# Attention half heads before a three-pass MLP: zeros products in the prologue, four q and k buffers, and the half heads' normalising and copying exchanged between ScalarE and VectorE

## The reference, cut to what matters

```python
# attention: B, H, S, D = 4, 8, 576, 64, causal window of 128 keys, ALiBi slope 2**-(h+1)
scores = scale * np.matmul(q, k.transpose(0, 1, 3, 2))
scores = np.where(mask, scores + bias[None], -1000000000.0)
scores = scores - np.max(scores, axis=-1, keepdims=True)
attn = np.exp(scores)
attn = attn / (np.sum(attn, axis=-1, keepdims=True) + 1e-09)
x = np.matmul(attn, v)                        # heads side by side: (4, 576, 512)
# block 1
xn = (x - mu) / np.sqrt(var + 1e-06) * g_ln
x = x + np.maximum(xn @ w_ch1, 0.0) @ w_ch2   # 512 -> 2048 -> 512
# block 2
h = np.maximum(x @ w_in, 0.0)                 # 512 -> 1024
h = h * (1.0 / (1.0 + np.exp(-conv_out)))     # conv_out: 3 taps over the sequence
out = h @ w_out
```

## Time and profile before

| | us |
|---|---|
| median of 3 runs | 871.1 (866.97 to 873.47) |
| the profiled execution | 875.55 |
| its span | 873.8 |
| PE busy | 828.9 (95%) |
| DVE, ACT, POOL busy | 525.8, 365.3, 177.2 |
| first 71.1 us: mean granted clock of TensorE | 0.64 |
| 71.1 to 136.0: the same | 0.79 |
| 182 to the end: the same | 0.99 or more |

### The profile page before, as it was taken

One profiled execution on the slowest core, in us unless ns is written; L12 is line 12 of the kernel. 1 busy time (PEld: TensorE's weight loads), 2 busy tenths in 40 slices (PEclk: granted clock), 3 DMA queues, 4 the chain that ended last, 5 costly groups with the idle time before them and its releaser, 6 DMA issues.

```text
span 873.8 us, 17079 instructions
## 1 busy us (share of the span) xinstructions
PE 828.9 (95%) x5836; PEld 778.6 (89%) x5836; DVE 525.8 (60%) x1444; ACT 365.3 (42%) x1007; POOL 177.2 (20%) x170
## 2 busy tenths in 40 slices
PE   8988878599998999999899999999999999999998
PEld 5556667589997999999899999999999899999998
DVE  3543455668755677764577773631226977888772
ACT  3423334356632365552255652221325444444432
POOL 6334456322201221110111120111111101111100
PEclk8558789999999999999999999999999999999999
DMA  4231343221203112301312311221222022211201
GB/s 125 63 93 55 92 134 93 82 66 51 82 8 116 54 44 69 96 9 55 99 35 63 96 42 56 77 68 43 89 85 83 14 84 75 75 56 46 81 21 41
DMA packets 56110, 59.29 MB, mean 68 GB/s; under 512 B 24800, under 2 KB 43232, under 8 KB 55520
## 3 DMA queue, kind: packets, MB, share of 16 engines
q1 hardware_dynamic: 56032, 58.30, 22.4%
HBM read 44.12 MB, written 14.16 MB: 67 GB/s over the span
## 4 chain that ended last, share of the span: by engine, by line
PE 78%; issue 9%; DVE 8%; ACT 2%; POOL 1%; SPq 1%; DMA 0%; ACTq 0%; POOLq 0%; DVEq 0%
PE bank L1280 21%; PE bank L1282 20%; PE bank L1281 20%; PE bank L1182 3%; PE bank L1206 3%; PE bank L1221 3%; PE bank L1251 3%; PE bank L1235 3%; PE bank L1195 2%; PE bank L1263 1%; PE bank L1173 1%; DVE small L905 1%; DVE prob L912 1%; DVE prob L949 1%; ACT prob L732 1%
## 5 line engine op out<-in xcount | busy, mean ns | idle before, releaser
L1280 PE MATMUL bank<-xn_hi,wa_hi 128*128 128x288 f32 x512 | 159.4, 311 | 3.6 <-DVE xn_lo L1001 2.4
L1280 PE MATMUL bank<-h_hi,wb_hi 128*128 128x288 f32 x512 | 158.4, 309 | 0.5 <-DVE ch_stage L1017 0.5
L1281 PE MATMUL bank<-xn_lo,wa_hi 128*128 128x288 f32 x512 | 154.0, 301 | 0.0
L1282 PE MATMUL bank<-xn_hi,wa_lo 128*128 128x288 f32 x512 | 153.8, 300 | 0.0
L1281 PE MATMUL bank<-h_lo,wb_hi 128*128 128x288 f32 x512 | 152.4, 298 | 0.0
L1282 PE MATMUL bank<-h_hi,wb_lo 128*128 128x288 f32 x512 | 152.1, 297 | 0.0
L1006 DVE SCALAR_TENSOR_TENSOR h_lo<-bank,h_hi 128x288 fp32r<-128x288 f32 x128 | 58.2, 454 | 123.2 <-ACT h_hi L762 121.8
L762 ACT ACTIVATE h_hi<-bank 128x288 fp32r<-128x288 f32 x128 | 52.4, 409 | 186.0 <-PE bank L1282 185.2
L1280 PEld LDWEIGHTS bank<-xn_hi,wa_hi 128*128 128x128 f32 x512 | 98.7, 193 | 7.2 <-issue 4.9
L1280 PEld LDWEIGHTS bank<-h_hi,wb_hi 128*128 128x128 f32 x512 | 97.7, 191 | 3.0 <-issue 1.4
L1281 PEld LDWEIGHTS bank<-xn_lo,wa_hi 128*128 128x128 f32 x512 | 98.9, 193 | 0.0
(11 more groups left out here) (127 smaller groups left out, 1721.8 us busy)
## 6 DMA issues: line engine op xcount, KB each, us to landing
w_stage<-w SPq DMA_DIRECT2D x32, 256.0 KB, 2.9
k_raw<-qkT SPq DMA_DIRECT2D x48, 144.0 KB, 2.9
q_raw<-qkT SPq DMA_DIRECT2D x48, 144.0 KB, 2.9
x_in<-x_spill SPq DMA_DIRECT2D x8, 580.0 KB, 4.2
ch_in<-ch_spill SPq DMA_DIRECT2D x8, 580.0 KB, 5.2
x_spill<-xT SPq DMA_DIRECT2D x4, 1152.0 KB, 4.6
ch_spill<-ch_stage SPq DMA_DIRECT2D x32, 144.0 KB, 1.9
out<-out_stage SPq DMA_DIRECT2D x32, 144.0 KB, 1.8
```

The costliest lines, as they stand in the source:

```text
L1280: nc.tensor.matmul(dst, w_h, a_h, start=start, stop=False)
L1281: nc.tensor.matmul(dst, w_h, a_l, start=False, stop=False)
L1282: last = nc.tensor.matmul(dst, w_l, a_h, start=False, stop=stop)
```

## The change

It does five things.

- **Zeros products.** The 14 at the start become 9. The fours before three heads go; instead 8 stand before the first HP, 4 before each of the six after it, 7 and 10 around the last heads, then 9 before the first OUT, 4 before the second and the third, and 4 before the first product of block 1: 79 instead of 44.
- **Four q and k buffers.** Two more buffers of 2x384 columns lie in the former gaps behind `half_pt0` and `half_pt1`. The loads of heads 2 and 3 are issued at the start, in front of the v loads of heads 1 and 2; each later one waits for the scores of head e - 4.
- **Pads later.** The new buffers lie where the pads of `pt_hi` and `pt_lo` are, so POOL clears these only after the last scores of half 1, in "first", and PE waits for them before the first O of batch 1 and no longer before "first".
- **Normalising on ACT, copying on DVE.** `half_normalise` is now on ACT, a Copy with a scale per row; DVE keeps the sum and the reciprocal as `half_inverse`, and takes `half_pt_copy`.
- **Other times.** In "first" HP comes at 2.2 slots after HS (2.9 before) and HO at 4.3 (5.15 before); the new steps have delays counted from HS. Head 0 of half 1 is normalised between the prologue and "first".

```diff
@@ -88,16 +88,18 @@
-HALF_FIRST = {("HS", 0): 0.0, ("HP", 0): 2.9, ("HO", 0): 5.15}
+HALF_FIRST = {("HS", 0): 0.0, ("HP", 0): 2.2, ("HO", 0): 4.3}
-WARM_START, WARM_HEAD, WARM_NORM = 14, 4, 6
+WARM_START = 9
+WARM = [(1.79, 8)] + [(m + 0.78, 4) for m in range(2, H)] + [(H + 0.3, 4), (H + 0.7, 3), (H + 1.2, 4), (H + 1.7, 6)]
+WARM += [(H + 2.3 + t, n) for t, n in ((0.3, 9), (0.6, 4), (0.9, 4), (1.2, 4))]
...
@@ -158,7 +160,7 @@
-        out += [(n - 0.2, ("WARM", WARM_HEAD)) for n in range(3)] + [(H + 2.3 + t, ("WARM", WARM_NORM)) for t in (0.3, 0.6, 0.9)]
+        out += [(t, ("WARM", n)) for t, n in WARM]
...
@@ -286,9 +288,10 @@
-        sb("half_gap0", [P, PTN - 512], scope=half)
+        half_qk2 = sb("half_qk2", [P, 2, 384], scope=half)
-        sb("half_gap1", [P, PTN - 512 + 2 * S + NT * D], scope=half)
+        half_qk3 = sb("half_qk3", [P, 2, 384], scope=half)
+        sb("half_gap1", [P, 2 * S + NT * D], scope=half)
...
@@ -299,6 +302,8 @@
+        half_qk += [half_qk2[0:D], half_qk3[0:D]]
+        assert PTN - 512 == 768
...
@@ -438,12 +443,12 @@
-                if e >= 2:
-                    c2, h2 = divmod(e - 2, H)
-                    sp.wait_ge(bank_filled, use_of(0, ("HS", c2, h2, len(HGROUPS[c2]) - 1)) + 1)
+                if e >= 4:
+                    c4, h4 = divmod(e - 4, H)
+                    sp.wait_ge(bank_filled, use_of(0, ("HS", c4, h4, len(HGROUPS[c4]) - 1)) + 1)
-                sp.dma_start(half_qk[e % 2][:, :, 0:n], qkT[0, h, :, :, HK0[c]:HK0[c] + n]).then_inc(half_qk_loaded[e % 2], 16)
+                sp.dma_start(half_qk[e % 4][:, :, 0:n], qkT[0, h, :, :, HK0[c]:HK0[c] + n]).then_inc(half_qk_loaded[e % 4], 16)
...
@@ -500,8 +505,10 @@
+            load_half_qk(0, 2)
+            load_half_qk(0, 3)
...
@@ -514,7 +521,7 @@
-                        e = half_no(a[0], a[1]) + 2
+                        e = half_no(a[0], a[1]) + 4
...
@@ -607,10 +614,13 @@
-            nc.gpsimd.memset(pt_hi[:, PTZA:PTN].bitcast(F32), 0.0).then_inc(zeros_ready, 1)
-            nc.gpsimd.memset(pt_lo[:, PTZA:PTN].bitcast(F32), 0.0).then_inc(zeros_ready, 1)
+            def clear_pt_pads():
+                pool.wait_ge(bank_filled, use_of(0, ("HS", 1, H - 1, 0)) + 1)
+                nc.gpsimd.memset(pt_hi[:, PTZA:PTN].bitcast(F32), 0.0).then_inc(zeros_ready, 1)
+                nc.gpsimd.memset(pt_lo[:, PTZA:PTN].bitcast(F32), 0.0).then_inc(zeros_ready, 1)
...
@@ -649,13 +659,15 @@
-                          ("W", 0.3, "w_lo"), ("Y", 1.0, "y"), ("HS", -early, "scale")]
+                          ("W", 0.3, "w_lo"), ("Y", 1.0, "y"), ("HS", -early, "scale"), ("HS", 0.9, "pads")]
+                    elif name == "pads" and a[0] == 1 and a[1] == H - 1:
+                        clear_pt_pads()
...
@@ -714,13 +726,13 @@
-            def half_pt_copy(c, h):
-                e = half_no(c, h)
-                act.wait_ge(bank_filled, use_of(0, ("HP", c, h, 0)) + 1)
-                if e >= 2:
-                    c2, h2 = divmod(e - 2, H)
-                    act.wait_ge(bank_filled, use_of(0, ("HO", c2, h2, 0)) + 1)
-                nc.scalar.activation(half_pt[e % 2][:], bank[bank_of(0, ("HP", c, h, 0))][:], ACT.Copy).then_inc(half_pt_ready, 1)
+            def half_normalise(c, h):
+                e, r = half_no(c, h), half_rows(c, h)
+                act.wait_ge(half_sum, 2 * e + 2)
+                for t in range(HNT[c]):
+                    rows, _, _, keys, _, col = HTILES[c][t]
+                    probs = half_prob_of(c, h)[0:rows, col:col + keys]
+                    nc.scalar.activation(probs, probs, ACT.Copy, scale=row_inv[0:rows, r + t:r + t + 1]).then_inc(half_prob, 1)
...
@@ -787,7 +799,7 @@
-                          ("HS", 0.5, "half_exps"), ("HP", 0.6 if kind == "prologue" else 0.3, "half_pt")]
+                          ("HS", 0.5, "half_exps"), ("HS", 1.85 if kind == "prologue" else 1.1, "half_normalise")]
...
@@ -823,6 +836,7 @@
+            half_normalise(1, 0)
...
@@ -899,17 +913,20 @@
-            def half_normalise(c, h):
+            def half_inverse(c, h):
-                dve.wait_ge(half_sum, 2 * e + 2)
-                for t in range(n):
-                    rows, _, _, keys, _, col = HTILES[c][t]
-                    probs = half_prob_of(c, h)[0:rows, col:col + keys]
-                    nc.vector.tensor_scalar(probs, probs, row_inv[0:rows, r + t:r + t + 1], None, ALU.mult).then_inc(half_prob, 1)
+            def half_pt_copy(c, h):
+                e = half_no(c, h)
+                dve.wait_ge(bank_filled, use_of(0, ("HP", c, h, 0)) + 1)
+                if e >= 2:
+                    c2, h2 = divmod(e - 2, H)
+                    dve.wait_ge(bank_filled, use_of(0, ("HO", c2, h2, 0)) + 1)
+                nc.vector.tensor_copy(half_pt[e % 2][:], bank[bank_of(0, ("HP", c, h, 0))][:]).then_inc(half_pt_ready, 1)
...
@@ -1038,17 +1055,20 @@
-                d_half = -0.3 if kind == "prologue" else -0.45
+                d_half = 1.78 if kind == "prologue" else 1.0
-                          ("HS", 0.3, "half_min"), ("HP", d_half, "half_normalise"), ("HO", 0.45 if kind == "prologue" else 0.3, "half_x")]
+                          ("HP", 0.45 if kind == "prologue" else 0.3, "half_pt"), ("HS", 0.3, "half_min"), ("HS", d_half, "half_inverse"), ("HO", 0.45 if kind == "prologue" else 0.3, "half_x")]
-                    elif name == "half_normalise":
-                        half_normalise(a[0], a[1])
+                    elif name == "half_inverse":
+                        if a[2] == len(HGROUPS[a[0]]) - 1 and not (kind == "prologue" and a[0] == 1):
+                            half_inverse(a[0], a[1])
+                    elif name == "half_pt":
+                        half_pt_copy(a[0], a[1])
...
@@ -1081,6 +1101,7 @@
+            half_inverse(1, 0)
...
@@ -1241,6 +1262,8 @@
+                    if is_int(batch) and batch == 1 and h == 0:
+                        pe.wait_ge(zeros_ready, 9)
...
@@ -1341,7 +1364,6 @@
-            pe.wait_ge(zeros_ready, 9)
```

15 lines of the change are left out of this document (8 added, 7 removed).

## The result

The changed kernel has a median of 842.28 us (839.82 to 845.15, 4 runs), the kernel before 871.8 (866.97 to 873.47, 4 runs with those shown ahead): 0.9671 of it, 95% interval 0.9615 to 0.9728. The forecast was 843. The profiled execution took 845.15 us, the slowest of the four, with a span of 843.4 and a mean clock of 0.99; before it was 0.95.

A forecast was written before the change was run, and what follows sets the result against it. PE was taken as the bound, at half clock in the prologue and waiting at HPs in "first". Gains 2.0 + 7.9 + 0.9 + 1.3 + 16.3 = 28.4 from 871.1 gave 843 us, range 834 to 853 (0.52).

The forecast's parts named there:

- The clock of the prologue: Prologue: the added zeros products bring granted clock from 0.50 to near 1.00, from about 15 us to its end.
- the slower rival: Zeros products don't hold the prologue's clock and each costs 0.44 us; rounds 7.2 us, total 884 us; chance 0.05.
- the reading of activity as occupied time: Old prologue would already run at high clock, making the 35 added products pure cost: 881 us; counted with the slower case.
- Rounds: Prologue, first to sixth HP: five rounds of 4.4 us, 22.0 instead of 29.9, gain 7.9 us.
- the stall s = 1.1: Prologue rounds: the add's stall beside POOL, between 0 and 2.8 us, taken as 1.1 on a 3.3 us loop.
- Start: Program start to first HP: it comes near 15.0 us instead of 17.03, gain 2.0; eight zeros products take 2.3.
- Last heads and normalisation: End of prologue: sixth HP to IN gains 0.9 us, IN to the first product gains 1.3 us.
- IN near 47: Profile sign: IN comes near 47 us, the first product of block 1 between 54 and 62.
- First: Stage "first", first product to last HP: 51.2 us against 67.5, a head every 6.6 us, gain 16.3.
- The add waits for a gap of POOL: Stage "first": this heads the chain over ACT and POOL that binds a head at 6.6 us, above PE's 5.5.
- The waits under 6 us in total: Profile sign in "first": PE's waits at HP total under 6 us, and these are on ACT.
- the rival with a moved wait: Stage "first": the add's stall delays the next head's minima, a head stays near 8 us; total 857 us; chance 0.20.

The follow-up runs named there:

- the run without the 70: The changed kernel with its 9 zeros products at the start and the 70 behind them left out; 849.25 us, ratio 0.9748 to the kernel before.

## Why the prediction was right, point by point

*The clock of the prologue.* Right, and by the reason given. The old prologue was occupied and slow, and the zeros products turned it; without them 95% of occupied time gave 0.50 again. That also settles the slower rival, and the reading of activity as occupied time with it: by "TensorE: Matmul & The Clock Gate" of the Trainium skill, Part 1, read so, the run without the 70 should have been at 1.00 and faster, and its row has 0.50 and 5.54 us per round. What in the zeros products does it is open: they are 512 columns wide, on all 128 rows and of type float32r, where the scores, transposes and outputs beside them are narrower and float32. No run takes these apart.

*Rounds.* 4.05 us measured against 4.4. PE's own sum of 4.0 was right; the stall s = 1.1 was not there. In the prologue the add of three columns took 0.295 us in the mean of seven. The copy of 512 columns on DVE took 0.69 (0.65 predicted; all 16 between 0.680 and 0.692), three Copies on ACT 1.15 (1.2). The loop had room, so the gain was 9.0. It had room with the old engines too (4.06 us in the run of the zeros products alone), so the prologue owes nothing to the exchange.

*Start.* 0.6 against 2.0. The step that failed is "I take the lower, since wide products are what raised the clock before": the eight took 3.6 us, the upper end, and in no execution with nine at the start did they take 2.3 (2.9 to 3.6, from start to start). The term also rests on one execution of each kernel: the run with the normalisation one place earlier, whose code is that of before up to there, had its first HP at 15.71, not 17.03, and the kernels with nine had it between 13.89 and 16.45. A difference of 2 us cannot be told from that. With 14 first, three traces agree within 0.2 us on a first HP about 3 us ahead of the profile after; that the whole kernel is faster by it is not shown, since the intervals (0.958 to 0.9662 and 0.9615 to 0.9728) overlap.

*Last heads and normalisation.* 0.7 and 1.4 against 0.9 and 1.3. The line "IN near 47" was a slip: by the prediction's own terms it is 15 + 22 + 13.3 = 50.3, and it came at 50.88. The first product, at 59.49, fell into its range.

*"First".* The mechanism was right, the size was not: 21.9 against 16.3. "The add waits for a gap of POOL" does happen, 2.88 us in one head, but it was taken for the length of a head, and it isn't: PE's own work is, forecast as 5.5 and measured as 5.40. Six heads at 5.40 instead of 6.6 are 7.2 us more than forecast, 4.5 instead of 5.0 to the first HP another 0.5, and the last head with its 8.73 took back 2.1. The prediction let every head meet a POOL run; but five of the eight adds took 1.22 us or less, and where two took 2.84 and 2.88, the HP was late enough. Part of the 21.9 is also the profile of before: 6.3 us of its 67.5 were gone in the run of the zeros products alone, as low clock. The waits under 6 us in total came out as 2.35, at one HO, and that one for DVE, not ACT: the last head's minima stood behind a low part of q.

```profile
97.42 1.51 DVE L1054 SCALAR_TENSOR_TENSOR q_st<-q_raw,q_st 64x576 fp32r<-64x576 f32 x1 [1.81 <-ACT q_st L707]
...
99.33 0.41 DVE L910 CUSTOM_DVE_ANT_0 prob<-bank,dist 128x256 f32<-128x256 f32 x1
```

It took twice its 0.76 beside POOL, and it came late because ACT had made the high part of q behind the Copies that waited for the add of 2.88. Without the add it came earlier and took 4.22, and PE's wait was the same. So the rival with a moved wait was right in kind, at one head, and wrong in size. What it needs is a long run of POOL, which only the seventh head meets, where the preparation of batch 1 begins. "SBUF — State Buffer", "Who interferes with whom", in the Trainium skill lets the two engines shut each other out for the length of an instruction; the rows agree (2.88 us under POOL's instructions), and show more, that DVE's add got no turn between instructions of POOL that stood back to back, for up to 7.22 us. That the steps moved "both escape the stall" is right too: all copies L929 took 0.69.

*Behind "first".* The prediction had no term here, and the profile after lost 3.1 us. About 1 us of it is the place of the cut: with HP 0.7 slots earlier, more of PE's work stands behind the last HP. Cut at the scores of batch 1, "first" won 20.9 and the part behind lost 725.2 - 723.0 = 2.2. In both kernels PE waits 3.9 us for a normalisation and then runs at half clock for a while; in the profile after a second such stretch followed:

```profile
124.00:126.00 2.00, 1.91 (x9) 1.88 (x10) 1.93 (x6) 1.15 (x2) 2.00 (x3) 0.50 0.00 0
...
138.00:140.00 2.00, 2.00 (x11) 2.00 (x11) 1.29 (x7) 0.02 (x1) 0.62 (x1) 0.50 0.00 0
```

It went on from about 137.4 to 140.9. From the transposes at 136.73 to the next waited scores at 143.70 are 6.97 us, and 5.43 before and in the kernel with 14 at the start, so it cost 1.5 us. That kernel has the same waits in the same order, and its clock was 1.00 from 128 to 138 us, where the stretch would lie. A third one, behind the normalisation at 244 us, lasted 6.8 us instead of 3.4 and cost the other 0.6. So the 2.2 us are low clock that came in one execution and not in the other, with the same waits.

*What the total owes to.* That 843 and 842.3 agree so closely is in part luck: in the profiles, which are both slower than their medians (by 3.8 and 2.9 us), "first" gave 5.6 more than forecast, the rounds 1.1 more, the start 1.4 less, and the part behind 3.1 less. Split by the runs, in us from the ratios times 871: the order of the half heads' work on DVE 16.8 (0.0193), the zeros products 6.7 (0.9748 - 0.9671) to 7.3 (0.0084), the buffers 3.9, the exchange of engines 4.4. The last two are differences of ratios whose intervals overlap. For the exchange the trace speaks, 2.3 us in "first"; for the buffers it shows 4.1 us at the first product and none at the end. The zeros products and the buffers also lean on each other: the zeros alone left a wait of 6.07 us that the buffers take away.

## What to carry to other kernels

A stage in which PE is busy 95% is not done with until its granted clock has been read: here 51 us of full work ran at half pace, and products of zeros, whose result nobody reads, paid for themselves. When an engine waits once per step for a chain over others, look first at the order in which that chain's instructions stand; one number in the order's table brought more than the exchange of engines, which paid at one head only. A DVE instruction that POOL shuts out costs what it delays on the bound engine, not its own length (2.88 us cost nothing at the HP behind it, 7.22 cost 3.95), and in these rows its length is that of POOL's run: a look at what ends POOL's run says more than the stall itself.

## What was not expected of the hardware

Scores, outputs and transposes alone, with PE busy 95% for 38 us, left the clock at 0.50 until the prologue was over, while with two products of 128x512 in a round of 3.6 us it was 1.00. Their data are all zeros, and the clock rose all the same.

The clock column reads 1.00 in the first microseconds of a program in which the work goes at the pace of 1.2 GHz: in the profile after the eighteen scores from 5.66 us took 7.27, in the kernel with 14 at the start 4.02, and this row covers the end of the slow part:

```profile
14.00:18.00 4.00, 4.00 (x14) 2.98 (x13) 0.27 (x1) 0.50 (x3) 2.52 (x3) 1.00 0.84 207
```

The eight zeros products up to 16.45 went at 0.45 us each in it. At the start the pace of known work is to be read and not the column.

An addition on 128x2 numbers, 0.16 us at its shortest, took 2.88 us under three POOL instructions back to back and 7.22 under eight, and ended each time within 0.02 us of POOL's run. The run can stop itself: in the profile after POOL's next input stood on ACT behind work that waited for the shut-out add, and the stall ended there. Reciprocals (0.17) and copies from a bank (0.69) kept their usual times beside the same runs. Without the add the next instruction from SBUF to SBUF, the low part of q, took 4.22 instead of 0.76: the stall was passed on, not removed. The two kinds differ: POOL's two clearings, which only write, held up the add (91.44 to 98.66, they ran from 97.55 to 98.64) and not the low part of q, which has two inputs in SBUF.
